# A fused attention and two-layer kernel on one core: the variance product of a unit, in two halves, next to the next unit's first coarse scores, and the first transposed probabilities next to the second coarse transposes

## The reference, cut to what matters

```python
mu = np.mean(x, axis=-1, keepdims=True)
var = np.mean((x - mu) ** 2, axis=-1, keepdims=True)
xn = (x - mu) / np.sqrt(var + 1e-06) * g_ln
ch = np.maximum(xn @ w_ch1, 0.0) @ w_ch2          # 512 -> 2048 -> 512
x = x + ch
...
k = np.maximum(xk @ w_k, 0.0)                      # 512 -> 1024
v = k * k @ w_v
r = 1.0 / (1.0 + np.exp(-(xr @ w_r)))
out = r * v
```

## Time and profile before

| what | value |
|---|---|
| median of 3 executions | 768.91 us (768.64 to 769.99) |
| the profiled execution's own time | 768.95 us |
| its span | 767.2 us |
| TensorE matmul busy | 747.5 us (97%) |
| VectorE, ScalarE, GpSimd busy | 57%, 36%, 29% |
| mean granted TensorE clock | 0.988 |

### The profile page before, as it was taken

The page is one execution under the profiler, slowest core; times in us unless marked ns, Lnnn a source line. Parts: engine busy times, 40 slices in busy tenths (PEclk is TensorE's granted clock), DMA queues, the critical chain, the costliest instruction groups (busy, mean ns, idle before and its releaser), DMA issues.

```text
span 767.2 us, 15782 instructions
## 1 busy us (share of the span) xinstructions
PE 747.5 (97%) x6412; PEld 690.5 (90%) x6412; DVE 437.9 (57%) x815; ACT 275.4 (36%) x656; POOL 225.7 (29%) x260
## 2 busy tenths in 40 slices
PE   5699999999999999999999999999999999999998
PEld 4499999999999999999999999998888888888886
DVE  5885773444654354655354332567686675766655
ACT  5655523223233233233233231456334434333322
POOL 5166763132444213345223222004111111111101
PEclk9689999999999999999999999999999999999999
DMA  9982441220441121251011003612003011010010
GB/s 183 229 295 54 89 87 42 48 63 11 84 98 37 24 45 56 53 109 41 14 25 41 14 1 128 241 56 86 1 1 110 0 48 36 1 56 1 0 56 28
DMA packets 118103, 49.67 MB, mean 65 GB/s; under 512 B 96656, under 2 KB 107152, under 8 KB 118032
## 3 DMA queue, kind: packets, MB, share of 16 engines
q1 hardware_dynamic: 118032, 48.68, 24.7%
HBM read 39.20 MB, written 9.45 MB: 63 GB/s over the span
## 4 chain that ended last, share of the span: by engine, by line
PE 95%; DVE 3%; ACT 1%; issue 1%; POOL 0%; DVEq 0%; POOLq 0%; ACTq 0%
PE psH L1014 27%; PE psY L1031 26%; PE psH L1065 13%; PE psY L1086 13%; PE psA L1047 6%; PE psA L948 2%; PE psA L917 2%; PE psA L865 1%; PE psA L893 1%; PE psA L928 1%; PE psA L878 1%; PE psA L854 0%; PE psA L953 0%; DVE prob_first L1403 0%; DVE xc_lo L1527 0%
## 5 line engine op out<-in xcount | busy, mean ns | idle before, releaser
L1014 PE MATMUL psH<-xc_hi,w_hi 128*128 128x288 f32 x512 | 155.9, 305 | 2.4 <-DVE xc_lo L1527 2.4
L1031 PE MATMUL psY<-h_hi,w_hi 128*128 128x288 f32 x512 | 153.0, 299 | 0.0
L1014 PE MATMUL psH<-xc_lo,w_hi 128*128 128x288 f32 x512 | 151.9, 297 | 0.0
L1014 PE MATMUL psH<-xc_hi,w_lo 128*128 128x288 f32 x512 | 151.8, 297 | 0.0
L1658 DVE SCALAR_TENSOR_TENSOR h_lo<-psH,h_hi 128x288 fp32r<-128x288 f32 x128 | 58.3, 455 | 163.5 <-ACT h_hi L1351 163.0
L1031 PE MATMUL psY<-h_lo,w_hi 128*128 128x288 f32 x512 | 150.7, 294 | 0.0
L1031 PE MATMUL psY<-h_hi,w_lo 128*128 128x288 f32 x512 | 150.7, 294 | 0.0
L1351 ACT ACTIVATE h_hi<-psH 128x288 fp32r<-128x288 f32 x128 | 52.5, 410 | 247.8 <-PE psH L1014 247.2
L839 POOL TENSOR_TENSOR relu_k<-relu_k 128x512 f32<-128x512 f32 (+1 forms) x39 | 38.7, 993 | 243.7 <-ACT relu_k L1313 243.7
L1014 PEld LDWEIGHTS psH<-xc_hi,w_hi 128*128 128x128 f32 x512 | 97.0, 189 | 5.8 <-issue 4.6
L1031 PEld LDWEIGHTS psY<-h_hi,w_hi 128*128 128x128 f32 x512 | 96.0, 188 | 1.7 <-issue 1.3
(11 more groups left out here) (179 smaller groups left out, 1344.2 us busy)
## 6 DMA issues: line engine op xcount, KB each, us to landing
w_raw<-in_moe_w_ch_dram SPq DMA_DIRECT2D x8, 1024.0 KB, 7.4
v_win<-in_v_dram SPq DMA_DIRECT2D x84, 56.0 KB
x_scratch<-x SPq DMA_DIRECT2D x8, 576.0 KB, 3.5
out_dram<-gate SPq DMA_DIRECT2D x17, 256.0 KB, 2.3
raw<-in_q_dram SPq DMA_DIRECT2D x112, 36.0 KB, 2.0
raw<-in_k_dram SPq DMA_DIRECT2D x96, 36.0 KB, 2.0
v_raw<-in_v_dram SPq DMA_DIRECT2D x12, 288.0 KB
x_sh<-x_scratch SPq DMA_DIRECT2D x3, 1026.0 KB, 5.7
```

Of the source, the lines that this page charges most:

```text
L1014: ins = mm(psH[:, m % 2, 0:N], ws[a][:, kt, f * P:(f + 1) * P], xx[bb][:, kt], start=(kt == 0 and i == 0), stop=(kt == KT - 1 and i == 2))
L1031: ins = mm(psY[:, d, 0:N], ws[a][:, f, d * P:(d + 1) * P], hs[bb][:, m % 2], start=(f == 0 and i == 0), stop=(f == NF1 - 1 and i == 2))
```

## The change

Two pieces are moved, and one is cut differently.

- `V` of units 1 to 7 goes from slot 0 to slot 2, right before `Sd` part 0 of the next unit, and shares the pair with it: it no longer fits in one bank beside `Sd`, so it is two halves of 144 columns, one in each bank from column 288 on. The two matmuls of 288 columns become four of 144. `Sd` part 0 is not held back by `V`. VectorE reads `V` only when this `Sd` is done, so that it doesn't read the banks while TensorE writes them.
- `PT` part 0 goes from slot 13 to slot 10, right after `PdT` part 1, and shares the pair with it (columns 288 on, two of the four transposes in each bank). ScalarE copies `PdT` part 1 only when this `PT` is done. `S` part 1 goes from slot 11 to slot 12.

```diff
--- before.py
+++ after.py
@@ -71,19 +71,19 @@
 
     SLOTS = 2 * NF1
     LEAD = 24
-    LATER = [(2, "Sd", 0), (5, "S", 0), (5, "Sd", 1), (8, "PdT", 0), (10, "PdT", 1), (11, "S", 1),
-             (13, "PT", 0), (15, "OD", 0), (15, "AV", 0), (19, "PT", 1), (19, "PT", 2), (21, "AV", 1), (24, "M", 0)]
+    LATER = [(2, "Sd", 0), (5, "S", 0), (5, "Sd", 1), (8, "PdT", 0), (10, "PdT", 1), (10, "PT", 0), (12, "S", 1),
+             (15, "OD", 0), (15, "AV", 0), (19, "PT", 1), (19, "PT", 2), (21, "AV", 1), (24, "M", 0)]
 
     TOGETHER = {("S", 1): (1, 2), ("AV", 1): (1, 2), ("OD", 0): (0, 1)}
 
 
     OTHERS = 4 * GU
-    SECOND = [("Sd", 1), ("AV", 0), ("PT", 2)]
+    SECOND = [("Sd", 1), ("PT", 0), ("AV", 0), ("PT", 2)]
 
     def parts_of(kind, u, n):
         return TOGETHER.get((kind, n), (n,)) if u else (n,)
 
-    OWN = [(0, "V", 0)]
+    OWN = [(2, "V", 0)]
 
     OWN_FIRST = [(2, "V", 0)]
 
@@ -93,10 +93,10 @@
     TURN = {"Tk": [(0, 1), (2, 3), (4, 5)], "Tq": [(0,), (1, 2)]}
 
     later = []
+    for u in range(NU):
+        later += [(SLOTS * u + s, kind, u, n) for s, kind, n in (OWN if u else OWN_FIRST)]
     for u in range(1, NU):
         later += [(SLOTS * (u - 1) + s + (BEHIND if u == 1 else 0), kind, u, n) for s, kind, n in LATER]
-    for u in range(NU):
-        later += [(SLOTS * u + s, kind, u, n) for s, kind, n in (OWN if u else OWN_FIRST)]
     later.sort(key=lambda x: x[0])
     steps = [x[0:3] for x in FIRST] + [x[1:] for x in later]
     place_of = {(kind, u, part): i for i, (kind, u, n) in enumerate(steps) for part in parts_of(kind, u, n)}
@@ -401,7 +401,12 @@
 
         def shares(i):
 
-            return steps[i][1] >= 1 and (steps[i][0], steps[i][2]) in SECOND
+
+            return steps[i][1] >= 1 and (steps[i][0], steps[i][2]) in SECOND or steps[i][1] >= 2 and steps[i][0::2] == ("Sd", 0)
+
+        def halves(tile):
+
+            return tile[:, :, OTHERS:OTHERS + N // 2]
 
         def wait_bank_out(eng, i):
 
@@ -489,7 +494,12 @@
 
         def turned_bank(i):
 
-            return pairs[pair_at(i)][0:RB + KB, int(shares(i)), 0:KT * ROWS]
+            kind, u, n = steps[i]
+            if u and n == 0:
+
+                return pairs[pair_at(i)][0:RB + KB, :, OTHERS:OTHERS + KT // 2 * ROWS]
+            bank = int(shares(i))
+            return pairs[pair_at(i)][0:RB + KB, bank:bank + 1, 0:KT * ROWS]
 
         def vw_slot(w):
             return vw_first[:, w] if w < NW_U else v_win[:, (w - NW_U) % 2]
@@ -924,8 +934,10 @@
                 pe.wait_ge(normed, w + 1)
                 wait_bank_out(pe, i)
                 p = prob_slot("S", u, n)[0:ROWS]
+                dst = turned_bank(i)
+                nj = dst.shape[2] // ROWS
                 for j in range(KT):
-                    ins = nc.tensor.transpose(turned_bank(i)[:, j * ROWS:(j + 1) * ROWS],
+                    ins = nc.tensor.transpose(dst[:, j // nj, j % nj * ROWS:(j % nj + 1) * ROWS],
                                               p[:, 2 * j * RB:2 * j * RB + RB + KB], ident[0:ROWS, 0:ROWS])
                 ins.then_inc(pt_done, 1)
 
@@ -967,13 +979,17 @@
             def variance(u):
                 i = place_of["V", u, 0]
                 wait_bank_out(pe, i)
-                dst = pairs[pair_at(i)][:, 0, 0:N]
                 if u == 0:
                     pe.wait_ge(sq_summed, 1)
-                    mm(dst, ones[:], xs[:, 0], start=True, stop=True).then_inc(var_done, 1)
-                else:
-                    pe.wait_ge(sum_lo_made, 2 * u)
-                    ones_by_sums(dst).then_inc(var_done, 1)
+                    mm(pairs[pair_at(i)][:, 0, 0:N], ones[:], xs[:, 0], start=True, stop=True).then_inc(var_done, 1)
+                    return
+                pe.wait_ge(sum_lo_made, 2 * u)
+                dst = halves(pairs[pair_at(i)])
+                for a in range(2):
+                    at = slice(a * (N // 2), (a + 1) * (N // 2))
+                    mm(dst[:, a], ones_r[:], sum_hi[:, at], start=True, stop=False)
+                    ins = mm(dst[:, a], ones_r[:], sum_lo[:, at], start=False, stop=True)
+                ins.then_inc(var_done, 1)
 
             def attend(slot):
                 for kind, u, n in steps_at(slot):
@@ -1181,6 +1197,9 @@
                 i = place_of["PdT", u, n]
                 act.wait_ge(pdt_done, 2 * u + n + 1)
                 act.wait_ge(av_done, count_by("AV", u))
+                if u and n == 1:
+
+                    act.wait_ge(pt_done, NW_U * u + 1)
                 copy(turned_place("PdT", u, n)[0:GU, 0:8 * GU].rearrange("p (a c) -> p a c", a=2), pairs[pair_at(i)][0:GU, :, 0:4 * GU]).then_inc(pdt_out, 1)
 
             def pt_o(u, n):
@@ -1193,7 +1212,8 @@
                     act.wait_ge(x2_made, KT * (u - 1))
                 elif u == 0 and n == 2:
                     act.wait_ge(od_done, 1)
-                copy(turned_place("PT", u, n)[0:RB + KB, 0:KT * ROWS], turned_bank(i)).then_inc(pt_out, 1)
+                src = turned_bank(i)
+                copy(turned_place("PT", u, n)[0:RB + KB, 0:KT * ROWS].rearrange("p (a c) -> p a c", a=src.shape[1]), src).then_inc(pt_out, 1)
 
             def od_o(u, n):
                 i = place_of["OD", u, n]
@@ -1531,8 +1551,16 @@
 
                 i = place_of["V", u, 0]
                 dve.wait_ge(var_done, u + 1)
-                src = pairs[pair_at(i)][0:W, 0, 0:N].rearrange("p (y a) -> p a y", a=NW_U)
-                chain(nc.vector.tensor_tensor(diag[0:W], src, ident[0:W, 0:W].unsqueeze(1).to_broadcast([W, NW_U, W]), ALU.mult))
+                if u == 0:
+                    src = pairs[pair_at(i)][0:W, 0, 0:N].rearrange("p (y a) -> p a y", a=NW_U)
+                    chain(nc.vector.tensor_tensor(diag[0:W], src, ident[0:W, 0:W].unsqueeze(1).to_broadcast([W, NW_U, W]), ALU.mult))
+                else:
+                    if u + 1 < NU:
+
+                        dve.wait_ge(sd_done, 2 * (u + 1) + 1)
+                    src = halves(pairs[pair_at(i)])[0:W].rearrange("p b (y a) -> p a b y", a=NW_U)
+                    eye = ident[0:W, 0:W].rearrange("p (b y) -> p b y", b=2).unsqueeze(1).to_broadcast([W, NW_U, 2, W // 2])
+                    chain(nc.vector.tensor_tensor(diag[0:W].rearrange("p a (b y) -> p a b y", b=2), src, eye, ALU.mult))
                 if u >= 1:
                     dve.wait_ge(rstd_made, u)
                 chain(nc.vector.tensor_reduce(var_e[0:W], diag[0:W], AX_X, ALU.add))
```

## The result

The changed kernel takes **771.6 us** (median of 6, 771.15 to 772.53) against 768.75 before (median of 6, 768.51 to 769.99): ratio 1.0031, 95% interval 1.002 to 1.0041. It is slower by 2.85 us by the medians, by 2.4 us by the ratio (interval 1.5 to 3.2). The forecast was 769.4, with a range of 768.0 to 773.3. The range held the time; the forecast's own case, no change, did not come true.

A forecast was written before the change was run, and what follows sets the result against it. The prediction took TensorE's own stream, busy for 97% of the span, to bound the kernel. Its terms, +1.2 - 0.4 - 0.3 = +0.5 us on 768.95, gave 769.45, forecast as 769.4 us, range 768.0 to 773.3.

The forecast's parts named there:

- the forecast's own case: Whole kernel: 769.4 us, 0.06% more, which a measurement can't tell from no change; chance 60%.
- rival 1: Narrow variance matmuls run at the plain fp32 rate: +0.72 us in each of 7 units, 773.2 us, slower; chance 22%.
- Rival 2: Narrow variance matmuls: short load and matmul don't overlap, 0.18 us each, 771.4 us, slower; chance 8%.
- Rival 4: A new wait, local scores for the exponential or first transposes for GpSimd: +3.5 us, 772.9 us; chance 5%.
- What bounds the kernel: In the eight units only TensorE's own stream counts: what a change takes out or adds, or waits it opens or closes.
- Variance product: Four matmuls of 144 columns at 0.12 us, 0.53 to the coarse scores against 0.36: +0.17 a unit, +1.2 us.
- The lower bound (columns alone): Narrow variance matmuls priced by width only, 0.073 us each: +0.03 a unit, +0.2 us.
- The wait on `sum_lo` in unit 1: TensorE's wait before unit 1's variance product goes, as the product comes two slots later: -0.4 us, once.
- The joined transposes: First local transposes behind the coarse ones save 0.04 us for each of 7 units: -0.3 us (0 to -0.6).
- What moves on the other engines, at nothing: Work shifted on VectorE, ScalarE and GpSimd costs nothing, each shift hidden by a margin.
- The two margins that I read: At least 0.5 us left before the next local scores; 0.7 us to spare at the first transposes for GpSimd's scaling.

The follow-up runs named there:

- experiment 1: The changed kernel with only the variance product moved and halved, `PT` part 0 and `S` part 1 in their old slots: 769.63 us, ratio 1.0006.
- experiment 2: The kernel before with only `PT` part 0 and `S` part 1 moved, `V` as before: 771.17 us, ratio 1.0028.
- experiments 5 and 6: The kernel before with the variance product of units 1 to 7 in its old slot, cut into halves (769.96 us) or into quarters of 72 columns (773.86 us).
- experiment 7: The changed kernel with GpSimd's first summing of batch 1's values in unit 0 in slot 20 instead of 18: 770.77 us, ratio 1.0018.

## Why the prediction was right in its range and wrong in its number

- **The range**: that it held the time is partly luck. What I counted gave 768.0 to 770.5 by itself; it reached 773.3 for rivals 1, 2 and 4, of which none came true as it was told.
- **What bounds the kernel**: right. Every term that moved the time did it through a wait or a distance on TensorE.
- **Variance product**, forecast +0.17 us a unit: measured +0.14 in the trace after (0.49 or 0.50 against 0.36), and +0.16 from C to D in experiment 1. The price of 0.12 was the load's 0.11, and for the first of the four 0.06; the last distance was 0.21 where I took 0.17, so two errors partly cancel. The lower bound (columns alone) and rival 1 (plain fp32 rate) fall by experiments 5 and 6. Rival 2 named a price near the total, 771.4, but by a mechanism that isn't there: the distances are 0.11, not 0.18, so load and matmul do overlap.
- **The wait on `sum_lo` in unit 1**, forecast -0.4: measured -0.49 (experiment 1).
- **The joined transposes**, forecast -0.04 a unit: measured -0.04 (experiment 2).
- **What moves on the other engines, at nothing**: this is the step that failed, at one sentence, "What follows `S` part 1 has 7 slots instead of 8 until slot 19". The two margins that I read, at the next local scores and at the first transposes, held: in unit 3 the exponential begins at 232.97 and the scores come at 235.58 without a wait. But for `S` part 1 I counted slots and read no row. In the first unit, where GpSimd and VectorE both split weights, the shift of one slot puts GpSimd's scaling, its summing and its weight pieces in one nearly unbroken stretch, and VectorE's weight piece against it. I had put this at nothing; it makes A to B 2.0 us longer, once.
- **Rival 4** was of the right kind, a new wait, and 5% was too little. Its price was 0.5 us in each of 7 units at a place that I named; the true one is 2 us in one unit at another place.

The sum with what was measured: 0.14 x 7 - 0.49 - 0.04 x 7 + 2.3 (the two waits, from experiment 7) - 0.2 (the wait ahead of `S` part 1) = +2.3 us, against 2.85 by the medians and 2.4 by the ratio, whose interval is 1.5 to 3.2.

The Trainium skill ("SBUF — State Buffer", section "SBUF: two separate sides") describes a port pair of which VectorE, with two SBUF inputs, and GpSimd each take hold for a whole instruction, whoever starts first, while the other is blocked. Experiment 7 agrees in direction: the one that starts first makes the other long. The section doesn't say who comes next. Here VectorE stood through the operation of GpSimd that was under way at its start and the three behind it.

## What to carry to other kernels

When a step is moved, follow its helpers to the fullest stretch of the program, not to a steady one, and read the rows there: seven units can be at peace and the first one pay for all. Where two engines slow each other, what counted here was which operations met, so busy shares said nothing (before, VectorE 22.77 and GpSimd 24.86 of the 34 us from 60.5 to 94.5); look at the longest single instruction of a kind against its shortest. And before a piece is cut to fit a bank, note that at 144 and at 72 columns a matmul cost its weight load, 0.11 us, so the cut cost time though no column was added.

## What the hardware showed that I had not expected

- VectorE's `w_lo` with the same shape took 0.70 to 4.57 us, by how it met GpSimd's operations.
- A rounded fp32 matmul with 128x128 weights costs 0.13 us at 288 columns, 0.12 at 256, and 0.11 at 144 and at 72. The first narrow one behind a wide one costs 0.06 to 0.07 at 144 columns and 0.04 at 72.
- Behind such short matmuls the second wide one comes late too, by 0.09 us after eight quarters and by 0.05 after four halves.
